# Unsplit attention scores beside the first chunk, scores of reversed sign, and other start addresses of the first layer's operands

## The chip, the cores and the metric

One NeuronCore of one Trainium2 chip. TensorE (PE in the profile, PEld its weight loads) multiplies, VectorE (DVE) and ScalarE (ACT) do everything elementwise, GpSimd (POOL) builds masks and issues transfers, SyncE (SP) issues the transfers of weights and output. The metric is the device time in microseconds (us) of one launch.

## The reference

Windowed attention with four sink keys, then two feed-forward layers on the same 1536 tokens:

```python
scores = scale * np.matmul(q, k.transpose(0, 1, 3, 2))        # batch 2, 8 heads, 768 positions, head size 64
keep = is_sink | in_window                                    # 4 sink keys, window of 128
scores = np.where(keep, scores, -1000000000.0)
scores = scores - np.max(scores, axis=-1, keepdims=True)
a = np.exp(scores)
a = a / (np.sum(a, axis=-1, keepdims=True) + 1e-09)
out = np.matmul(a, v)                                         # becomes x, 1536 x 512
h = x @ w_in                                                  # 512 x 2048
g = np.where(h >= 1, h, np.where(h <= -1, 0.0, (h + 1) ** 2 / 4))
x = g @ w_out                                                 # 2048 x 512
h = x @ w_in2
g = np.where(h > 0.0, h, np.exp(np.minimum(h, 0.0)) - 1.0)
y = g @ w_out2
```

All inputs and outputs are fp32; q and k are some 31 times larger than v, so the scores are large and the softmax is sharp.

## The kernel before

**Split operands.** A product that must be nearly exact in fp32 is made of operands rounded to TensorE's one-pass fp32 type (F32R) and their remainders: with `x_hi`, `x_lo`, `win_hi`, `win_lo` the first product of a layer is three matmuls (L510 to L512), and so is the second (L525 to L527). ACT makes a rounded part with a copy (CAST), DVE the remainder with a subtraction.

**Chunks.** The first layer runs over 6 chunks of 256 tokens, the second over 3 chunks of 512. A chunk has 16 tiles `t` of 128 hidden units. In tile `t` PE does `hidden(t)` (12 matmuls into `h_ps`), then `outward(t - 2)` (12 matmuls into `y_ps`); ACT and DVE make `ramp`, `g_full`, `g_hi` and `g_lo` from `h_ps`. In a first-layer matmul the moving operand (x or g) has 256 columns.

**Attention.** Chunk 0's attention is done first, alone (the `first_*` functions), in plain fp32. After that the attention of chunk c+1 is done beside the first layer of chunk c: the table BESIDE puts the scores of heads 0 to 7 at the ends of tiles 2, 3, 5, 6, 8, 9, 11 and 12, the exponentials one tile later, the transposes two tiles later, and the values of a pair of heads three tiles after its second head. For every head, ACT copies `k_hi` and `q_parts` (L596, L597), DVE subtracts `k_lo` and the low half of `q_parts` (L787, L788), and only then PE may run the four score matmuls (L463, L464), which wait for the semaphore qk_lo_ready. In `q_parts` the upper 64 rows hold the rounded q and the lower 64 its remainder, so a matmul with 128 rows covers both. DVE adds the mask and takes the maximum (L800), negates it (L803), and ACT uses that as the bias of the exponential (L606). DVE then normalises (L808 to L814), PE transposes the probabilities (L473, L479), ACT copies them (L611), and PE multiplies by the values (L493, L495).

**Weights.** The first layer's 16 pieces of weights are split once: three while the first attention runs (SPLITS_ALONE), the other thirteen beside chunk 0, piece 3+t at the end of tile t, each by one ACT copy (L647) and one DVE subtraction (L845) of 1024 columns. The second layer's weights are split beside chunk 5 and the first second-layer chunk.

**Order.** Every engine works through its own instruction list in order, and semaphores join them. Within a tile DVE does: the remainder split of this tile's head, the normalising of the last one, `g_lo`, `g_full`, the maximum, the sinks' split, the weights' split. POOL issues the loads of q and k of head h once the head two before it has been split (L378), which frees the buffer.

**Where things lie.** Tiles in SBUF are placed one behind the other. All that stands ahead of `small` is a multiple of 256 bytes long, `small` is 64 bytes and `half` 128. The change's title counts from a line of 256 bytes; by those sizes x begins 64 bytes into a line, and so does g, in the kernel before. The weights begin 128 bytes into one, the second layer's x and g 192.

Of the kernel before, what the change touches and what calls it, by code (L numbers as in the profile page):

```python
# [26 lines left out]
ALU = mybir.AluOpType  # L27
ACT = mybir.ActivationFunctionType

P = 128  # L30
# [21 lines left out]
LOWEST = -3.0e38  # L52
# [29 lines left out]
def build(nc, qk_first, v_first, q_t, k_t, v_w, v_s, w_in, w_out, ident_d, out, n_sink, window):  # L82
# [8 lines left out]
    with ExitStack() as ctx:  # L91
# [50 lines left out]
        behind = sb("behind", [P, 64])  # L142
# [11 lines left out]
        first_scores, first_max, first_neg_max, first_exp = sem("first_scores"), sem("first_max"), sem("first_neg_max"), sem("first_exp")  # L154
        first_sum, first_inv, first_probs, first_probs_t = sem("first_sum"), sem("first_inv"), sem("first_probs"), sem("first_probs_t")
        first_copied, first_attn = sem("first_copied"), sem("first_attn")
        qk_loaded = [sem(f"qk_loaded{n}") for n in range(4)]
        v_loaded = [sem("v_loaded0"), sem("v_loaded1")]
# [10 lines left out]
        max_done, neg_max_ready, sum_done, inv_ready, probs_ready = sem("max_done"), sem("neg_max_ready"), sem("sum_done"), sem("inv_ready"), sem("probs_ready")  # L169
# [40 lines left out]

        def begins(c, n):

            return isinstance(c, int) and c == 1 and n == 0
# [117 lines left out]
        def _(pool):  # L331
# [40 lines left out]

            def load_head(c, h):
                if isinstance(c, int) and c == 1 and h < 2:

                    pool.wait_ge(first_scores, h + 2)
                else:
                    pool.wait_ge(qk_lo_ready, heads_before(c, h) - 1)  # L378
                for to, src in zip((ks[:, h % 2, :], qs[:, h % 2, :]), (k_t, q_t)):
                    pool.dma_start(to, src[bass.ds(heads_before(c, h), 1)].rearrange("o p n -> (o p) n")).then_inc(qk_loaded[h % 4], 16)  # L380
# [16 lines left out]
            load_head(1, 0)  # L397
            load_head(1, 1)
# [4 lines left out]
            for h in range(2, HEADS):  # L403
                load_head(1, h)
                if h > 2 * 2 and h % 2 == 1:
                    load_values(1, h // 2)
# [14 lines left out]
        def _(pe):  # L421
# [43 lines left out]

            def transposes(c, h):
                p, hh = h // 2, h % 2
# [3 lines left out]
                start = hh * (SW + NS)  # L471
                for n, (j, col) in enumerate(((0, start), (0, start + P), (1, start), (1, start + P))):
                    last = pe.transpose(t_ps[:, n * P:(n + 1) * P], probs[:, j, col:col + P], ident[:, :])  # L473
                last.then_inc(probs_t_ready, 1)
                if hh == 1:
# [56 lines left out]
            def layer_chunk(layer, c, attend=None):  # L532
                for t in range(FT):
# [3 lines left out]
                    if attend is not None:  # L537
# [4 lines left out]
                        for h in BESIDE[0][t]:  # L542
                            scores(attend, h)
# [23 lines left out]
        def _(act):  # L567
            def first_exponents(p):
                banks = flight[p % IN_FLIGHT][0]
                act.wait_ge(first_neg_max, p + 1)  # L570
                if p >= IN_FLIGHT:
                    act.wait_ge(first_probs_t, 2 * (p - IN_FLIGHT + 1))
                for hh in range(2):
                    for j in range(QB):
                        nc.scalar.activation(seen_probs(p, hh)[:, SEEN_OF[j]], banks[hh][:, SEEN_OF[j]], ACT.Exp,
                                             bias=tops[:, p % IN_FLIGHT, hh, j:j + 1],
# [14 lines left out]
            def split_head(c, h):  # L591

                act.wait_ge(qk_loaded[h % 4], (heads_before(c) // 4 + (h // 4 + 1)) * 32)
                if not begins(c, h):
                    act.wait_ge(scores_ready, heads_before(c, h) * QB)
# [3 lines left out]
            def exponent(c, h):  # L599
                p, hh = h // 2, h % 2  # L600
                if hh == 0 and not begins(c, p):
                    act.wait_ge(probs_t_ready, pairs_before(c, p) * 2)
                    act.wait_ge(sinks_t_ready, pairs_before(c, p))
                act.wait_ge(neg_max_ready, heads_before(c, h) + 1)
                for j in range(QB):
                    nc.scalar.activation(probs[:, j, hh * SW:(hh + 1) * SW], s_ps[j][:, 0:SW], ACT.Exp, bias=top[:, hh, j:j + 1],  # L606
                                         accum_out=total[:, hh, j:j + 1]).then_inc(exp_done, 1)
# [377 lines left out]
```

## Time and profile before

| what | us |
|---|---|
| three runs | 638.13, 638.5, 640.57 |
| median | 638.5 |
| the profiled execution's own time | 640.01 |
| its span, first to last instruction | 638.3 |
| its granted clock | 1.000 (the upper level, 2.4 GHz) |
| PE busy / DVE busy / ACT busy | 618.0 / 339.7 / 387.9 |
| POOL busy | 74.4 |

The profiled execution is 1.5 us above the median of the runs and 1.7 us above its own span. Times in the rows count from the first instruction. Of that span the first 24.0 us are the attention of chunk 0, 24.0 to 371.1 the first layer's six chunks, and the rest the second layer. "Idle before" is the time in which an engine stood still ahead of an instruction, with the instruction that ended it. Matmuls overlap, so the length of one says little; the distance from one start to the next is its price.

### The profile page before, as it was taken

To read this page: it belongs to the slowest core of one execution; us is meant where nothing else is said; L and a number is where in the kernel's file an instruction comes from. 1 tells how busy PE (TensorE), PEld (TensorE's weight loads), DVE (VectorE), ACT (ScalarE), POOL (GpSimd) and SP (SyncE) were. 2 spreads that over 40 slices of the span, in tenths; PEclk is the share of its full clock that TensorE was granted. 3 is DMA by queue.
4 is the path that set the end of the run, shared out by engine and by line. 5 is a ranking of instruction groups with operands and counts; after the bars stand their busy time and mean duration, and the time that the engine had idled before them with its cause. 6 is when DMAs were issued, how large, how long until landed. Compare 5 with 4: busy or idle time off the path is not lost.

```text
span 638.3 us, 12201 instructions
## 1 busy us (share of the span) xinstructions
PE 618.0 (97%) x4164; PEld 552.0 (86%) x4164; DVE 339.7 (53%) x899; ACT 387.9 (61%) x926; POOL 74.4 (12%) x147
## 2 busy tenths in 40 slices
PE   5799999999999999999999999999999999999997
PEld 3688899999999999999999988888888888888886
DVE  6799958766775677487646653222332222322221
ACT  5888877776886787787767764333443334533333
POOL 5213212221221223023000000000000000000000
PEclk9999999999999999999999999999999999999999
DMA  8664212320321222123054500000100000100001
GB/s 280 223 217 142 81 41 66 106 67 27 102 89 40 64 89 89 40 64 104 0 192 145 193 1 0 2 0 1 66 0 0 0 1 1 66 0 0 0 0 66
DMA packets 15276, 42.49 MB, mean 67 GB/s; under 512 B 2852, under 2 KB 4536, under 8 KB 15248
## 3 DMA queue, kind: packets, MB, share of 16 engines
q0 software_dynamic: 7040, 20.57, 10.5%
q1 hardware_dynamic: 8208, 21.56, 9.7%
q8 instruction: 15, 0.25, 0.1%
q14 instruction: 13, 0.11, 0.1%
HBM read 38.98 MB, written 3.15 MB: 66 GB/s over the span
## 4 chain that ended last, share of the span: by engine, by line
PE 85%; DVE 7%; ACT 4%; issue 2%; DMA 0%; ACTq 0%; SPq 0%; DVEq 0%
PE h_ps L510 13%; PE h_ps L512 12%; PE h_ps L511 12%; PE y_ps L525 9%; PE y_ps L527 9%; PE y_ps L526 9%; PE s_ps L525 3%; PE s_ps L527 3%; PE s_ps L526 3%; PE o_ps L493 3%; PE t_ps L473 2%; DVE wout_lo L845 1%; PE s_ps L463 1%; PE s_ps L464 1%; DVE win_lo L845 1%
## 5 line engine op out<-in xcount | busy, mean ns | idle before, releaser
L510 PE MATMUL h_ps<-x_hi,win_hi 128*128 128x256 f32 (+1 forms) x576 | 185.7, 322 | 0.8 <-DVE g_full L869 0.3
L512 PE MATMUL h_ps<-x_hi,win_lo 128*128 128x256 f32 (+1 forms) x576 | 182.3, 317 | 0.0
L511 PE MATMUL h_ps<-x_lo,win_hi 128*128 128x256 f32 (+1 forms) x576 | 181.6, 315 | 0.0
L525 PE MATMUL y_ps<-g_hi,wout_hi 128*128 128x256 f32 (+1 forms) x480 | 145.8, 304 | 1.8 <-DVE g_lo L858 1.8
L527 PE MATMUL y_ps<-g_hi,wout_lo 128*128 128x256 f32 (+1 forms) x480 | 144.9, 302 | 0.0
L526 PE MATMUL y_ps<-g_lo,wout_hi 128*128 128x256 f32 (+1 forms) x480 | 144.3, 301 | 0.0
L510 PEld LDWEIGHTS h_ps<-x_hi,win_hi 128*128 128x128 f32 x576 | 108.3, 188 | 9.3 <-DVE g_full L869 1.2
L512 PEld LDWEIGHTS h_ps<-x_hi,win_lo 128*128 128x128 f32 x576 | 108.8, 189 | 8.4
L511 PEld LDWEIGHTS h_ps<-x_lo,win_hi 128*128 128x128 f32 x576 | 108.3, 188 | 8.0
L873 DVE SCALAR_TENSOR_TENSOR g_full<-g_full,h_ps 128x512 f32<-128x512 f32 x48 | 33.0, 687 | 151.9 <-ACT g_full L680 151.9
L858 DVE TENSOR_TENSOR g_lo<-g_full,g_hi 128x256 fp32r<-128x256 f32 (+1 forms) x144 | 73.7, 512 | 52.9 <-ACT g_hi L665 52.2
L678 ACT ACTIVATE ramp<-h_ps 128x512 f32<-128x512 f32 x48 | 28.7, 597 | 117.5 <-PE h_ps L512 116.9
L665 ACT CAST g_hi<-g_full 128x256 fp32r<-128x256 f32 (+1 forms) x144 | 68.4, 475 | 50.2 <-DVE g_full L873 34.1
L525 PEld LDWEIGHTS y_ps<-g_hi,wout_hi 128*128 128x128 f32 x480 | 90.2, 188 | 7.1 <-DVE g_lo L858 1.4
L527 PEld LDWEIGHTS y_ps<-g_hi,wout_lo 128*128 128x128 f32 x480 | 90.9, 189 | 4.2
L526 PEld LDWEIGHTS y_ps<-g_lo,wout_hi 128*128 128x128 f32 x480 | 90.2, 188 | 4.0
L869 DVE SCALAR_TENSOR_TENSOR g_full<-h_ps,ramp 128x256 f32<-128x256 f32 x96 | 40.3, 420 | 21.4 <-ACT ramp L675 21.3
L606 ACT ACTIVATE probs<-s_ps,small 128x260 f32<-128x260 f32 x80 | 37.3, 470 | 20.3 <-DVE small L803 20.3
L673 ACT ACTIVATE ramp<-h_ps,half 128x256 f32<-128x256 f32 x96 | 45.4, 473 | 5.3 <-PE h_ps L512 4.8
L380 POOL DMA_DIRECT2D ks<-in_k x40 | 22.1, 551 | 207.5 <-DVE q_parts L788 205.8
L675 ACT ACTIVATE ramp<-ramp 128x256 f32<-128x256 f32 x96 | 40.1, 418 | 3.0
L525 PE MATMUL s_ps<-g_hi,wout_hi 128*128 128x512 f32 x96 | 37.8, 394 | 0.0
(110 smaller groups left out, 814.3 us busy)
## 6 DMA issues: line engine op xcount, KB each, us to landing
ks<-in_k POOLq DMA_DIRECT2D x40, 260.0 KB, 2.9
raw<-in_w_in SPq DMA_DIRECT2D x11, 512.0 KB, 4.0
raw<-in_w_out SPq DMA_DIRECT2D x11, 512.0 KB, 4.1
qs<-in_q POOLq DMA_DIRECT2D x40, 128.0 KB, 2.8
vals<-in_v POOLq DMA_DIRECT2D x20, 192.0 KB, 3.0
out_y<-xy SPq DMA_DIRECT2D x12, 256.0 KB, 2.1
xy<-in_w_in SPq DMA_DIRECT2D x5, 512.0 KB, 5.2
xy<-in_w_out SPq DMA_DIRECT2D x5, 512.0 KB, 4.1
```

Of the source, the lines that this page charges most:

```text
L510: pe.matmul(o, win_hi[:, k, f], x_hi[:, k, :], start=(k == 0), stop=False)
L511: pe.matmul(o, win_hi[:, k, f], x_lo[:, k, :], start=False, stop=False)
L512: last = pe.matmul(o, win_lo[:, k, f], x_hi[:, k, :], start=False, stop=(k == KT - 1))
L525: pe.matmul(o, wout_hi[:, t, cols], g_hi[:, t % GR, :], start=begin, stop=False, skip_group_check=True)
L526: pe.matmul(o, wout_hi[:, t, cols], g_lo[:, t % GR, :], start=False, stop=False, skip_group_check=True)
L527: last = pe.matmul(o, wout_lo[:, t, cols], g_hi[:, t % GR, :], start=False, stop=(t == FT - 1), skip_group_check=True)
L606: nc.scalar.activation(probs[:, j, hh * SW:(hh + 1) * SW], s_ps[j][:, 0:SW], ACT.Exp, bias=top[:, hh, j:j + 1], accum_out=total[:, hh, j:j ...
L665: nc.scalar.copy(g_hi[:, t % GR, :], g_full[:, t % 2, :]).then_inc(g_hi_ready, 1)
L673: nc.scalar.activation(ramp[:, t % 2, :], h, ACT.Relu, bias=half[:, 0:1], scale=0.5).then_inc(ramp_ready, 1)
L675: nc.scalar.activation(ramp[:, t % 2, :], ramp[:, t % 2, :], ACT.Square).then_inc(bent_ready, 1)
L858: nc.vector.tensor_tensor(g_lo[:, t % GR, :], g_full[:, t % 2, :], g_hi[:, t % GR, :].bitcast(F32), ALU.subtract).then_inc(g_lo_ready, 1)
L869: nc.vector.scalar_tensor_tensor(g, h, 1.0, ramp[:, t % 2, :], ALU.max, ALU.min).then_inc(g_ready, 1)
```

## The change

Three things are changed.

1. Beside chunk 0, the attention (of chunk 1) is done in *units* in place of heads. A unit is one block of 128 queries (j) of both heads of a pair. Its scores are two plain fp32 matmuls with 64 rows each (`unit_scores`), straight from the loaded q and k; nothing is split. q and k come as pairs of heads (`in_q_pairs`, `in_k_pairs`), so four loads of q and four of k take the place of eight. The maximum, exponentials, normalising, transposes and copies are those of a head, with the roles of j and hh exchanged. Beside chunks 1 to 4 heads are split as before. ACT's and DVE's `split_head(1, 0)` ahead of chunk 0 is gone.
2. The scaled scores get the reversed sign: the reduction takes the minimum, the exponential has scale -1, and the instruction that negated the maximum (L765, L803) is gone, everywhere.
3. `half` is 32 bytes longer, and 192 bytes (`beyond_x`) lie between `x_lo` and `g_hi`: x now begins 96 bytes into a line of 256, g 32. `behind` grows by 256 bytes so that the second layer's x and raw weights still lie behind all of the first layer's tiles; their place in a line stays.

```diff
-        half = sb0("half", [P, 32])
+        half = sb0("half", [P, 40])
         x_hi, x_lo = sb0("x_hi", [P, KT, CT], F32R), sb0("x_lo", [P, KT, CT], F32R)
+        beyond_x = sb0("beyond_x", [P, 48])
...
-        behind = sb("behind", [P, 64])
+        behind = sb("behind", [P, 128])
...
+            def load_pair(p):
+                if p < 2:
+
+                    pool.wait_ge(first_scores, p + 2)
+                else:
+                    pool.wait_ge(qk_lo_ready, 2 * (p - 1))
+                for to, src in zip((ks[:, p % 2, :], qs[:, p % 2, :]), (k_pairs, q_pairs)):
+                    pool.dma_start(to, src[p]).then_inc(pair_loaded[p % 2], 16)
...
+            def unit_scores(c, u):
+                p, j = u // 2, u % 2
+                pe.wait_ge(pair_loaded[p % 2], (p // 2 + 1) * 32)
+                if not begins(c, u):
+                    pe.wait_ge(exp_done, heads_before(c, u) * QB)
+                for hh in range(2):
+                    dims = slice(HD * hh, HD * (hh + 1))
+                    pe.matmul(s_ps[hh][:, 0:SW], qs[dims, p % 2, j * P:(j + 1) * P], ks[dims, p % 2, j * SW:(j + 1) * SW],
+                              start=True, stop=True).then_inc(scores_ready, 1)
...
                 for h in BESIDE[0][t]:
-                    if h > 0:
+                    if h > 0 and not in_units(c):
                         split_head(c, h)
...
-            split_head(1, 0)
             layer_chunk(0, 0, 1, splits_first)
...
-                        nc.vector.tensor_tensor_reduce(seen, seen, mask[:, SEEN_OF[j]], SCALE, LOWEST, ALU.add, ALU.max,
+                        nc.vector.tensor_tensor_reduce(seen, seen, mask[:, SEEN_OF[j]], -SCALE, HIGHEST, ALU.add, ALU.min,
                                                        tops[:, p % IN_FLIGHT, hh, j:j + 1]).then_inc(first_max, 1)
-                dve.wait_ge(first_max, (p + 1) * 2 * QB)
-                at_once = tops[:, p % IN_FLIGHT, :, :]
-                nc.vector.tensor_scalar(at_once, at_once, -1.0, None, ALU.mult).then_inc(first_neg_max, 1)
```

PE's list in tile 5 of chunk 0, from the transposes of head 1 (unit 1) to the next tile's first matmul, before:

```order
L473 MATMUL t_ps<-ident,probs 128x128 [waits probs_t_copied,probs_ready]
L473 MATMUL t_ps<-ident,probs 128x128 x3
L479 MATMUL o_ps<-ident,probs 8x128 x2
L463 MATMUL s_ps<-k_hi,q_parts 128x260 [waits exp_done,qk_lo_ready]
L464 MATMUL s_ps<-k_lo,q_parts 128x260
L463 MATMUL s_ps<-k_hi,q_parts 128x260
L464 MATMUL s_ps<-k_lo,q_parts 128x260
L510 MATMUL h_ps<-x_hi,win_hi 128x256 [waits g_ready,w_lo_ready,w_hi_ready]
```

and the same place in the changed kernel:

```order
L502 MATMUL t_ps<-ident,probs 128x128 [waits probs_t_copied,probs_ready]
L502 MATMUL t_ps<-ident,probs 128x128 x3
L508 MATMUL o_ps<-ident,probs 8x128 x2
L492 MATMUL s_ps<-ks,qs 128x260 [waits exp_done,pair_loaded1]
L492 MATMUL s_ps<-ks,qs 128x260
L539 MATMUL h_ps<-x_hi,win_hi 128x256 [waits g_ready,w_lo_ready,w_hi_ready]
```

The four split matmuls are now two, and the wait for DVE's split has become a wait for the load.

DVE's list at the same place, from the weights' split at the end of tile 4 to the one at the end of tile 5, before:

```order
L845 TENSOR_TENSOR wout_lo<-xy,wout_hi 128x1024 [waits w_hi_ready]
L787 TENSOR_TENSOR k_lo<-ks,k_hi 128x520 [waits qk_hi_ready]
L788 TENSOR_TENSOR q_parts<-qs,q_parts 64x256
L858 TENSOR_TENSOR g_lo<-g_full,g_hi 128x256 [waits g_hi_ready]
L869 SCALAR_TENSOR_TENSOR g_full<-h_ps,ramp 128x256 [waits bent_ready]
L800 ISA s_ps,small<-s_ps,mask 128x260 [waits scores_ready]
L800 ISA small 128x1
L800 ISA s_ps,small<-s_ps,mask 128x260 [waits scores_ready]
L800 ISA small 128x1
L803 TENSOR_SCALAR small<-small 128x2 [waits max_done]
L820 TENSOR_TENSOR sinks_t<-o_ps,sinks_t 8x256 [waits sinks_hi_ready]
```

and in the changed kernel:

```order
L874 TENSOR_TENSOR wout_lo<-xy,wout_hi 128x1024 [waits w_hi_ready]
L887 TENSOR_TENSOR g_lo<-g_full,g_hi 128x256 [waits g_hi_ready]
L898 SCALAR_TENSOR_TENSOR g_full<-h_ps,ramp 128x256 [waits bent_ready]
L828 ISA s_ps,small<-s_ps,mask 128x260 [waits scores_ready]
L828 ISA small 128x1
L828 ISA s_ps,small<-s_ps,mask 128x260 [waits scores_ready]
L828 ISA small 128x1
L849 TENSOR_TENSOR sinks_t<-o_ps,sinks_t 8x256 [waits sinks_hi_ready]
```

The two subtractions between the weights' split and `g_lo`, and the negation behind the maxima, are gone.

## Rows read from the trace of the kernel before

**Rows 1.** The page's part 1: busy us, share of the span, instructions

```profile
PE 618.0 (97%) x4164; PEld 552.0 (86%) x4164; DVE 339.7 (53%) x899; ACT 387.9 (61%) x926; POOL 74.4 (12%) x147
```

**Rows 2.** Chunks 0, 1, 5: stretch, us, PE busy (x), clock, DMA share, GB/s

```profile
24.01:89.98 65.97, 61.42 (x510) 1.00 0.43 137
89.98:148.75 58.77, 58.44 (x510) 1.00 0.24 71
...
324.75:371.14 46.39, 45.70 (x387) 1.00 0.49 172
```

**Rows 3.** Waits of PEld in chunk 0 (24.01:89.98): us in total, times, longest

```profile
PEld s_ps L463 <- DVE q_parts L788: 5.4, 7, 1.3
...
PEld y_ps L525 <- DVE wout_lo L845: 0.6, 1, 0.6
```

**Rows 4.** Busy PE, PEld, DVE, ACT, POOL: three tiles of chunk 0, of chunk 1

```profile
46.55:60.05 13.50, 12.40 (x104) 11.39 (x104) 12.28 (x34) 11.95 (x31) 3.28 (x6) 1.00 0.47 157
...
109.65:121.34 11.69, 11.69 (x105) 11.20 (x104) 8.96 (x31) 9.34 (x28) 3.22 (x6) 1.00 0.31 90
```

**Rows 5.** Groups by form, 46.55 to 60.05: the split of a head, ACT then DVE

```profile
L596 ACT CAST k_hi<-ks 128x520 fp32r<-128x520 f32 x2 | 1.2, 624 | 0.0
...
L597 ACT CAST q_parts<-qs 128x256 fp32r<-128x256 f32 x2 | 0.8, 404 | 0.0
...
L787 DVE TENSOR_TENSOR k_lo<-ks,k_hi 128x520 fp32r<-128x520 f32 x2 | 1.4, 694 | 0.0
...
L788 DVE TENSOR_TENSOR q_parts<-qs,q_parts 64x256 fp32r<-64x256 f32 x2 | 0.8, 422 | 0.0
```

**Rows 6.** Timeline of PE in tile 5 of chunk 0: start us, us, instruction

```profile
41.83 0.38 PE L479 MATMUL o_ps<-ident,probs 128*8 128x128 f32 x2
43.13 0.39 PE L463 MATMUL s_ps<-k_hi,q_parts 128*128 128x260 f32 x1 [0.92 <-DVE q_parts L788]
```

**Rows 7.** Timeline of PE in chunk 4: scores after transposes, then values and scores

```profile
305.84 0.36 PE L463 MATMUL s_ps<-k_hi,q_parts 128*128 128x260 f32 x1
306.04 0.28 PE L464 MATMUL s_ps<-k_lo,q_parts 128*128 128x260 f32 x1
...
306.40 0.28 PE L510 MATMUL h_ps<-x_hi,win_hi 128*128 128x256 f32 x1
...
308.80 0.28 PE L525 MATMUL y_ps<-g_hi,wout_hi 128*128 128x256 f32 x1
...
309.23 1.09 PE L493 MATMUL o_ps<-probs_t,vals 128*64 128x256 f32 x12
310.25 0.39 PE L495 MATMUL o_ps<-sinks_t,vsink_parts 128*128 128x256 f32 x1
310.47 0.28 PE L463 MATMUL s_ps<-k_hi,q_parts 128*128 128x260 f32 x1
```

**Rows 8.** Timeline of PE, starts of matmuls: chunk 4, chunk 5, the second layer

```profile
307.10 0.28 PE L510 MATMUL h_ps<-x_hi,win_hi 128*128 128x256 f32 x1
...
310.94 0.28 PE L510 MATMUL h_ps<-x_hi,win_hi 128*128 128x256 f32 x1
...
344.93 0.28 PE L510 MATMUL h_ps<-x_hi,win_hi 128*128 128x256 f32 x1
...
351.99 0.28 PE L525 MATMUL y_ps<-g_hi,wout_hi 128*128 128x256 f32 x1
...
450.10 0.39 PE L510 MATMUL h_ps<-x_hi,win_hi 128*128 128x512 f32 x1
...
452.85 0.39 PE L525 MATMUL s_ps<-g_hi,wout_hi 128*128 128x512 f32 x1
```

**Rows 9.** Timeline at the first attention's first maximum

```profile
6.64 0.14 DVE L761 DVE_READ_ACCUMULATOR2_ANT small<- 128x1 f32 x1
...
7.12 0.37 ACT L575 ACTIVATE probs<-s_ps,small 128x128 f32<-128x128 f32 x1 [4.11 <-DVE small L765]
```

More of the change, by code:

```diff
@@ L51 @@
 MASKED = -1e9
-LOWEST = -3.0e38
+HIGHEST = 3.0e38
 SPLITS_ALONE = {0: [0], 1: [1], 2: [2]}
@@ L79, with build @@
 IN_FLIGHT = 2
-def build(nc, qk_first, v_first, q_t, k_t, v_w, v_s, w_in, w_out, ident_d, out, n_sink, window):
+def build(nc, qk_first, v_first, q_pairs, k_pairs, q_t, k_t, v_w, v_s, w_in, w_out, ident_d, out, n_sink, window):
     NS = n_sink
@@ L209, in pairs_before, with in_units, splits_before, parts_of @@
             return (c - 1) * PAIRS + p
+        def in_units(c):
+            return isinstance(c, int) and c == 1
         def begins(c, n):
-            return isinstance(c, int) and c == 1 and n == 0
+            return in_units(c) and n == 0
+        def splits_before(c, h):
+            return (c - 2) * HEADS + h
+        def parts_of(c, n):
+            return [(n % 2, hh) for hh in range(2)] if in_units(c) else [(j, n % 2) for j in range(QB)]
         size = KT * GW
@@ L402, in _ @@
             load_values(1, 1)
[L403 to L406, printed above, removed]
+            for p in range(2, PAIRS):
+                load_pair(p)
+                load_values(1, p)
             with pool.Fori(2, NC) as c:
@@ L470, in transposes @@
                     pe.wait_ge(probs_t_copied, heads_before(c, h))
-                start = hh * (SW + NS)
-                for n, (j, col) in enumerate(((0, start), (0, start + P), (1, start), (1, start + P))):
+                blocks = [(j, hh * (SW + NS) + block * P) for j, hh in parts_of(c, h) for block in range(2)]
+                for n, (j, col) in enumerate(blocks):
                     last = pe.transpose(t_ps[:, n * P:(n + 1) * P], probs[:, j, col:col + P], ident[:, :])
                 last.then_inc(probs_t_ready, 1)
-                if hh == 1:
+                if h % 2 == 1:
                     if not begins(c, p):
@@ L542, in layer_chunk @@
                         for h in BESIDE[0][t]:
-                            scores(attend, h)
+                            (unit_scores if in_units(attend) else scores)(attend, h)
                 outward(layer, c, FT - 2)
@@ L599, in exponent @@
             def exponent(c, h):
-                p, hh = h // 2, h % 2
-                if hh == 0 and not begins(c, p):
+                p = h // 2
+                if h % 2 == 0 and not begins(c, p):
                     act.wait_ge(probs_t_ready, pairs_before(c, p) * 2)
                     act.wait_ge(sinks_t_ready, pairs_before(c, p))
[L604 to L607, printed above, removed]
+                act.wait_ge(max_done, (heads_before(c, h) + 1) * QB)
+                for n, (j, hh) in enumerate(parts_of(c, h)):
+                    nc.scalar.activation(probs[:, j, hh * SW:(hh + 1) * SW], s_ps[n][:, 0:SW], ACT.Exp, scale=-1.0,
+                                         bias=top[:, h % 2, n:n + 1], accum_out=total[:, h % 2, n:n + 1]).then_inc(exp_done, 1)
             def copy_probs_t(c, h):
                 act.wait_ge(probs_t_ready, heads_before(c, h) + 1)
-                nc.scalar.copy(probs_t[:, h % 2, :], t_ps[:, :]).then_inc(probs_t_copied, 1)
+                if in_units(c):
+                    half_of_both = probs_t[:, :, h % 2 * 2 * P:(h % 2 + 1) * 2 * P]
+                    nc.scalar.copy(half_of_both, t_ps[:, :].rearrange("p (h n) -> p h n", h=2)).then_inc(probs_t_copied, 1)
+                else:
+                    nc.scalar.copy(probs_t[:, h % 2, :], t_ps[:, :]).then_inc(probs_t_copied, 1)
                 if h % 2 == 1:
@@ L811, in normalise @@
                 dve.wait_ge(inv_ready, heads_before(c, h) + 1)
-                for j in range(QB):
+                for n, (j, hh) in enumerate(parts_of(c, h)):
                     v = probs[:, j, hh * SW:(hh + 1) * SW]
-                    nc.vector.tensor_scalar(v, v, total[:, hh, j:j + 1], None, ALU.mult).then_inc(probs_ready, 1)
+                    nc.vector.tensor_scalar(v, v, total[:, h % 2, n:n + 1], None, ALU.mult).then_inc(probs_ready, 1)
             def split_sinks(c, h):
@@ L827, in before_layer @@
                 for h in BESIDE[0][t]:
-                    if h > 0:
+                    if h > 0 and not in_units(c):
                         split_head(c, h)
```

58 lines of the change are left out of this document (28 added, 30 removed).

## The prediction

> **What bounds the kernel now.** I read the page first, then the windows chunk by chunk, then the waits of PE's weight loads inside the one chunk that stands out, and last PE's timeline. The page says that PE is busy for 97% of the span, and DVE and ACT for 53% and 61% [rows 1]. So time can be won in three places only: where PE waits, in what PE is given to do, and in the distance from one matmul to the next. The windows show where it waits. Chunks 0 and 1 give PE the same 510 instructions, but chunk 0 takes 65.97 us and chunk 1 58.77 [rows 2]: 7.2 us of chunk 0 are waits. The waits view names them: 5.4 us in seven waits of the first score matmul for DVE's `q_parts` (L788), the longest 1.3, and 0.6 in one wait for DVE's `wout_lo` [rows 3]. The cause is in the windows of three tiles: beside chunk 0 DVE is busy for 12.28 of 13.50 us and ACT for 11.95, since they split weights too; beside chunk 1 the same three tiles take 11.69 us, PE is busy for all of them, and DVE has 8.96 and ACT 9.34 to do [rows 4]. DVE and ACT set the pace of chunk 0, PE that of the others. One such wait: the transposes' last part starts at 41.83, the scores behind it at 43.13 [rows 6], 1.30 later.
>
> **The change part by part.**
>
> *The splits of q and k beside chunk 0 go.* Per head that is 624 + 404 ns of ACT and 694 + 422 ns of DVE [rows 5]. Three tiles hold two heads: DVE's 12.28 us become 12.28 - 2 x 1.12 = 10.0, ACT's 11.95 - 2 x 1.03 = 9.9, against PE's 11.69 [rows 4]. Both are then below PE, and PE sets the pace of chunk 0 as in the others. What PE waited for, q_parts, isn't made any more: **-5.4 us** [rows 3]. The new wait is for the load of a pair. POOL issues pair 2 once units 0 and 1 have their maxima (tile 3) and pair 3 behind the values of pair 2, whose own wait ends in tile 6; they are needed in tiles 8 and 11, two tiles and more (over 7 us at 11.69 for three) later, so I cost it at nothing. Queued behind that wait on PE would be the whole next tile. Of the other 1.8 us of waits (7.2 - 5.4), the 0.6 for `wout_lo` comes from the same overload; the rest is the start of the chunk, where three engines go through ramp, g and the split of weights by turns, and stays. I take **-0.5**, between 0 and -1.
>
> *The scores' own price on PE.* Four split matmuls take 0.56 us from start to start where transposes stand ahead (305.84 to 306.40) and 0.47 behind values (310.47 to 310.94) [rows 7, 8]. Three of the eight heads are of the first kind. The trace has no fp32 matmul with 64 rows at the upper clock that stands alone; the nearest are the values, also plain fp32, also two side by side: twelve instructions, four of 256 columns and eight of 128, in 1.02 us (309.23 to 310.25) [rows 7]. In pairs that is 1024 columns, 1.0 ns each. A unit is four such instructions of 260 columns in pairs, 520 columns: 0.52. A change between plain fp32 and split matmuls costs time on both sides: from 308.80 to 309.23 there are three matmuls of 0.113 and 0.09 more, from 310.25 to 310.47 one and 0.11 more [rows 7]. So a unit costs between 0.52 and 0.72. Upper end: 5 x (0.72 - 0.47) + 3 x (0.63 - 0.56) = +1.5; lower end, no such edge anywhere: 5 x 0.05 - 3 x 0.04 = +0.1. I take **+0.9**, a little above the middle, because the values' rows show both edges each time.
>
> The Trainium skill, "FP8 and Floating Point Precision", section "TensorE Precision Notes", has true fp32 take four passes through the array; four of 260 columns at 2.4 GHz are 0.43 us a unit as an estimate, with which this term would be +0.2; the values' row (1.0 ns a column) speaks for more.
>
> *The pace behind the scores.* The same matmul has two paces. From 307.10 to 308.80 fifteen take 1.70 us, 113.3 ns each; from 344.93 to 351.99 sixty take 7.06, 117.7 ns each [rows 7, 8]. Nothing is waited for in either, and the clock is 1.00 in both [rows 2]. Followed through the timeline, the quick pace comes where a longer gap has stood behind plain fp32 transposes, the slow one behind split scores. Of the first layer's 2304 matmuls with 256 columns some 1200 run at the slow pace by their starts, among them all of chunk 5. In chunk 0 about 120 slow ones (five tiles of 24) follow scores alone; a unit ends like the transposes do, which would make them quick: 120 x 4.4 ns = 0.5. I take **-0.3**.
>
> *The reversed sign.* The negation of the first maximum lies on the way to the first exponential: 6.64 + 0.14 is the end of the maximum, 7.12 the start of ACT [rows 9]. Without it ACT starts some 0.3 earlier, and the first attention is a chain, so **-0.3** (0 to -0.7, if a later one counts as well). Beside the layers the negations are on DVE, which has 2.7 us to spare in three tiles [rows 4]: nothing, covered by PE's matmuls.
>
> *The new start addresses.* They touch every moving operand of the 2304 matmuls and so their pace, whose mean now is (1104 x 113.4 + 1200 x 117.7) / 2304 = 115.6 ns. If all become quick: 1200 x 4.4 ns = -5.3 us. If all become slow: 1104 x 4.4 = +4.9. The trace holds two other placings. The second layer's x and g begin 192 bytes into a line, and twelve matmuls of 512 columns take 2.75 us (450.10 to 452.85 [rows 8]), 114.6 ns for 256 columns. The scores' four moving blocks begin in four different places (k_hi 128 and 144 bytes into a line, k_lo 160 and 176), and take 0.47 for four of 260 columns, 117.5 each, 115.8 without the 1.7 ns of four columns at 2.4 GHz. The mean of these two is 115.2, or 2304 x -0.4 ns = **-0.9 us**; the ends -5.3 and +4.9 are kept.
>
> **Sum.** -5.4 - 0.5 + 0.9 - 0.3 - 0.3 - 0.9 = -6.5 us. On the profiled execution's own 640.0 that is 633.5; it stood 1.5 above the median, so against the median of 638.5 I forecast **632.0**.
>
> **The rivals.**
> - *The placing makes all matmuls quick* (-5.3 in place of -0.9): 627.6. For it: the quick pace is a stable one that the same instructions hold for whole tiles. Against: nothing says that 96 and 32 bring it about.
> - *The placing makes all slow* (+4.9): 637.8. For it: chunk 5, where nothing disturbs PE, runs slow throughout (46.39 us for 387 instructions, 120 ns each with its two gaps [rows 2]).
> - *The stalls only move.* DVE's 10.0 and ACT's 9.9 of 11.69 are busy time; each wait between them adds. If ACT and DVE again end last, at `g_lo` or `wout_lo` instead of q_parts, half of the 5.4 comes back: 634.7.
> - *Slower than before:* a start off the present grid may make a matmul dearer than either pace. The scores' second and third matmul, one of which begins 32 bytes past a multiple of 64 as x and g now will, stand 0.12 us apart (306.04 to 306.40 is three steps [rows 7]). At 120 ns for all 2304: 2304 x 4.4 = +10.1, less the other terms (-5.6): 643.0. It ends slower than before once a matmul costs over 2.4 ns more than now, 118.0.
> - *The steps drop to the floor:* with no loss between matmuls, 256 columns at 2.4 GHz are 106.7 ns; if the new places remove what makes 113 out of it, to halfway (110), 2304 x -5.6 = -12.9 instead of -0.9: 620.0. The Trainium skill, "TensorE: Matmul & The Clock Gate", section "Back-to-back issue gap", gives columns / 2.4 + 2.5 ns, 109.2 here, and by that this case would be 618.2. The trace disagrees at both paces and in the second layer.
>
> **How the numbers follow.** Forecast 0.42, all quick 0.25, all slow 0.15, stalls move 0.10, slower 0.05, floor 0.03. The likeliest gives 632.0, by itself 629.5 to 634.5. The range of 625 to 638 takes in the quick case with its own spread and the slow one, and leaves out the last two and the tails. A measurement of this kernel can tell some 0.5% (3.2 us) from no change: faster means below 635.3, slower above 641.7. Faster: nearly all of the forecast and the quick case, the floor, half of the moved stalls, 0.76; within: the slow case and the other half, 0.18; slower 0.06.
>
> **What would show each step.** Chunk 0's window should shrink from 65.97 to about 60; the waits there shouldn't name the scores, nor `ks` loads; DVE and ACT in three tiles of it should show some 10 us of 11.7. From the start of a unit to the next tile's first matmul there should be 0.5 to 0.75. The other chunks' windows change by the pace alone: 58.8 now, 56.8 if all is quick, 60 if slow, and chunk 5's 46.39 would fall to 44.8. The second layer (267 us) should stay. I am wrong if chunk 0 keeps over 63 us, or if chunk 1 moves by more than 2 us, where the addresses would outweigh everything else.

## The result and the profile after

In eleven executions of each kernel the changed one took 643.27 us in the median (641.02 to 649.91), the one before 638.5 (637.99 to 641.74): a ratio of 1.0065, 95% interval 1.0043 to 1.0087. The forecast was 632.0, in a range of 625 to 638: wrong in size and in sign. The profiled execution took 641.91 us, 1.9 more than that of before, and its span, 640.1 us, is 1.8 longer. The page's part 1, which answers to [rows 1]:

```profile
PE 624.7 (98%) x4164; PEld 556.0 (87%) x4164; DVE 324.9 (51%) x839; ACT 382.5 (60%) x910; POOL 69.1 (11%) x139
```

DVE lost 60 instructions and 15 us, as it should. ACT lost the 16 copies of the split, 8.2 us by [rows 5], but only 5.4 us of busy time: neighbours overlap in the profile, so an instruction's length isn't what its going saves. PE has as many instructions as before and is busy for 6.7 us more. Where, the windows tell (stretch, its length, PE busy with its matmuls, granted clock, DMA share, GB/s), of before the start, chunks 1 to 4 together and the second layer (chunks 0 and 5 are in [rows 2]), then of after the start, chunk 0, chunks 1 to 4, chunk 5 and the second layer.

```profile
0.00:24.01 24.01, 13.34 (x88) 1.00 0.75 261
...
89.98:324.75 234.77, 233.69 (x2035) 1.00 0.22 68
...
371.14:638.28 267.14, 263.84 (x1154) 1.00 0.03 12
```

```profile
0.00:24.37 24.37, 14.61 (x88) 0.93 0.77 263
24.37:87.73 63.36, 62.53 (x512) 1.00 0.35 115
87.73:326.27 238.54, 237.73 (x2035) 1.00 0.22 67
326.27:372.83 46.56, 45.89 (x387) 1.00 0.49 172
372.83:639.98 267.15, 263.94 (x1155) 1.00 0.03 12
```

Chunk 0 gave 2.6 us (some 5.5 to 6 were forecast), chunks 1 to 4, in which PE is given the same instructions and only start addresses and DVE's negations are changed, cost 3.8, chunk 5 (46.39 before [rows 2]) 0.2, the second layer nothing. The start has its own disturbance: its clock is 0.93.

The waits of PE's weight loads in chunk 0, all that reach 0.4 us (total, times, longest), against [rows 3]:

```profile
PEld h_ps L539 <- issue: 3.2, 10, 0.3
PEld o_ps L524 <- issue: 0.7, 4, 0.2
PEld s_ps L492 <- issue: 0.7, 3, 0.2
PEld y_ps L554 <- DVE wout_lo L874: 0.6, 1, 0.6
PEld y_ps L554 <- issue: 0.4, 1, 0.4
```

The 5.4 us for q_parts are gone, and none for a pair's load came. The 0.6 for `wout_lo` has stayed. What stands first now has no releaser and comes ten times, 0.3 us each: an edge between kinds of matmul, of which more below. Three tiles of chunk 0, with two units (busy PE, PEld, DVE, ACT, POOL), against [rows 4]:

```profile
43.30:55.88 12.58, 12.58 (x106) 11.08 (x104) 9.82 (x27) 10.53 (x27) 2.14 (x4) 1.00 0.52 174
```

DVE has 9.8 us to do (10.0 forecast), ACT 10.5 (9.9, from which the lengths of the splits had been taken in full), and PE sets the pace, busy for all 12.58. But 12.58 isn't the 11.69 of a chunk without splits: PE itself had more to do.

Where the extra time of chunks 1 to 4 is, PE's timeline shows. The first and the last of 24 layer matmuls of one tile in chunk 1:

```profile
128.66 0.28 PE L539 MATMUL h_ps<-x_hi,win_hi 128*128 128x256 f32 x1
...
131.38 0.28 PE L556 MATMUL y_ps<-g_hi,wout_lo 128*128 128x256 f32 x1
```

Those are 23 steps in 2.72 us, 118.3 ns each. Counted over all of chunks 1 to 4, the mean step from one layer matmul to the next was 115.5 ns before (quick and slow ones mixed) and is 118.1 now: 2.6 ns more on some 1480 such steps is the 3.8 us.

### The profile page after: what moved, and what is told of

It is laid out like the page before. It is cut to its first block, busy times and chain, and to the rows that moved or that the text cites. A ratio compares the mean times of both kernels' runs of the same rounds, so it can differ in the third digit from the quotient of the medians.

```text
span 640.1 us, 12174 instructions
## 1 busy us (share of the span) xinstructions
PE 624.7 (98%) x4164; PEld 556.0 (87%) x4164; DVE 324.9 (51%) x839; ACT 382.5 (60%) x910; POOL 69.1 (11%) x139
## 4 chain that ended last, share of the span: by engine, by line
PE 94%; ACT 2%; DVE 1%; issue 1%; DMA 0%; ACTq 0%; SPq 0%; DVEq 0%
PE h_ps L539 14%; PE h_ps L541 13%; PE h_ps L540 13%; PE y_ps L554 10%; PE y_ps L556 10%; PE y_ps L555 10%; PE s_ps L554 3%; PE s_ps L556 3%; PE s_ps L555 3%; PE o_ps L522 3%; PE t_ps L502 3%; PE s_ps L482 1%; PE s_ps L483 1%; PE o_ps L524 1%; PE s_ps L492 1%
## 5 line engine op out<-in xcount | busy, mean ns | idle before, releaser
L828 DVE CUSTOM_DVE_ANT_0 s_ps<-s_ps,mask 128x260 f32<-128x260 f32 x80 | 32.9, 453 | 10.9 <-PE s_ps L483 6.1
```

## The placing: the runs

**Each part alone.** Four runs on one chip: the change with the placing undone, the placing alone, the sign alone, and the change again. The kernel without the new starts:

```diff
-        half = sb0("half", [P, 40])
+        half = sb0("half", [P, 32])
-        beyond_x = sb0("beyond_x", [P, 48])
-        behind = sb("behind", [P, 128])
+        behind = sb("behind", [P, 64])
```

> The changed kernel with half, beyond_x and behind as they were, so that x and g begin 64 bytes into a line again; units and reversed sign stay. If the start addresses made the change slower (theory A), chunks 1 to 4 go back to 58.6 to 58.8 us from 59.5 to 59.7, chunk 0 stays near 63 or falls by up to 0.8, and the time is 3 to 4 us below the kernel before. If the units or the sign did it (theory B), chunks 1 to 4 stay at 59.5 to 59.7 and the time stays 1 to 5 us above before.

The kernel before with the opposite edit, `half` 40, `beyond_x` 48, `behind` 128:

> The kernel before with the three changed sizes alone: x 96 bytes into a line, g 32. Theory A: no first-layer matmul keeps the quick pace of 113.3 ns, chunks 1 to 4 take 59.5 to 59.7 us, and the time is 4 to 6 us above before. Theory B: chunks as before within 0.1 us and the time within 1 us.

The kernel before with the reversed sign only (the first attention's part of the edit; the later chunks' is the same):

```diff
-   nc.vector.tensor_tensor_reduce(seen, seen, mask[:, SEEN_OF[j]], SCALE, LOWEST, ALU.add, ALU.max,
+   nc.vector.tensor_tensor_reduce(seen, seen, mask[:, SEEN_OF[j]], -SCALE, HIGHEST, ALU.add, ALU.min,
...
-   nc.vector.tensor_scalar(at_once, at_once, -1.0, None, ALU.mult).then_inc(first_neg_max, 1)
...
-   bias=tops[:, p % IN_FLIGHT, hh, j:j + 1],
+   scale=-1.0, bias=tops[:, p % IN_FLIGHT, hh, j:j + 1],
```

> The kernel before with the reversed sign alone (minimum, scale -1, no negation). The first attention ends 0.3 us sooner by the changed kernel's first maximum; everything behind it as before: 638.2 us, between 637.8 and 638.6. If it costs something (the rival), the time is 1 us or more above before, and a window of the first 24 us or of chunk 0 shows it.

The changed kernel unedited:

> The changed kernel again, on the chip of the other three. Its eleven runs spread over 9 us with granted clocks of 0.992 to 1.000. If the spread is the clock in the first attention, this run's windows differ from the first profile's in the first 24 us alone (24.4 us at 0.93 there), and 24.0 or less is seen at clock 1.00; if it is the pace of matmuls, chunk windows differ by over 0.5 us.

Against the kernel before on the same chip (639.56 in 29 executions): units and sign at the old place 637.86, ratio 0.9953 (0.9928 to 0.9977); the placing alone 644.7, 1.0082 (1.0044 to 1.0119); the sign alone 638.47, 0.997 (0.9949 to 0.9992); the change 641.66, 1.0034 (1.0014 to 1.0054). So the parts have opposite signs, and the placing decides. The lowest time of each, at a clock of 0.999 or more, says the same: 637.93 before, 634.59, 643.69, 636.52, 640.79. By these the placing costs 5.8 on the one base and 6.2 on the other (5.1 and 3.8 by the medians). Chunks 0, 1 to 4 and 5 of the placing alone, and then of units and sign without it:

```profile
24.09:90.14 66.05, 61.87 (x510) 1.00 0.44 137
90.14:328.60 238.46, 237.63 (x2035) 1.00 0.23 67
328.60:375.15 46.55, 45.88 (x387) 1.00 0.50 171
```

```profile
25.71:89.10 63.39, 62.48 (x511) 0.98 0.36 112
89.10:323.72 234.62, 233.59 (x2035) 1.00 0.23 68
323.72:368.74 45.02, 44.11 (x387) 1.00 0.52 176
```

Chunks 1 to 4 take 238.5 with the new starts and 234.6 with the old, whatever else is in the kernel. In chunk 0 of the placing alone the loss is 0.1 us: DVE and ACT set the pace there, and a slower PE waits less (5.0 us for `q_parts` instead of 5.4). Once the splits are gone the placing costs in chunk 0 too. There the profile at the old place, run once more, has its first 2.5 us at half clock and then

```profile
27.90:88.59 60.69, 59.83 (x500) 1.00 0.34 108
```

which makes some 62.0 us for chunk 0 at full clock, an estimate, against 63.36 at the new place. Chunk 5 has two lengths at the old place, 46.3 to 46.4 (two profiles, [rows 2] one of them) and 44.9 to 45.0 (four); in the longer nearly all of its steps are slow, in the shorter nearly all are quick. With x at 96 and g at 32 only the longer comes up.

The sign alone did more than its place in the first attention. Its chunk 0, of which the first stretch ran at half clock:

```profile
24.87:90.23 65.36, 61.47 (x510) 0.98 0.43 132
...
24.87:27.60 2.73, 2.73 (x14) 0.50 0.53 175
```

At full clock that is some 64.0 us (an estimate: half of 2.73 less) for 65.97 before, and PE's loads wait 4.3 us for `q_parts` instead of 5.4. The reading, which no further run tests: with the splits still there DVE holds up chunk 0, and its negations cost time; without the splits it has time to spare, so this gain and that of the units are in part the same.

**Which start costs.** The places count, as above, from weights that begin 128 bytes into a line; what the runs show is the effect of each shift. All in the changed kernel, on one chip, one execution each (as built, x is at 96 and g at 32). x at 96 and g at 64 is `beyond_x` 56; x at 64 and g at 32 is `half` 32 and `beyond_x` 56; both at 0 is `half` 16, both at 128 is `half` 48, without `beyond_x`.

> The changed kernel, x 96 bytes into a line as changed, g back at 64. Chunks 1 to 4 took 238.5 us with x 96 and g 32, and 234.6 with both at 64. If the start of each moving operand acts on its own matmuls, this lies halfway, 236.5 (and the next run too, the two losses adding up to 3.9). If a matmul hands its phase on to the next, so that one kind of start is enough to end the quick pace for both, this and the next both stay at 238 to 238.5.

> The changed kernel, x back at 64 bytes, g at 32 as changed. Own effect: 236.5 us for chunks 1 to 4; handed on: 238 to 238.5.

> The changed kernel, x and g at the start of a line (0 and 0). If only multiples of 64 bytes matter, the two paces are as at 64: chunks 1 to 4 take 234.4 to 234.9 us, steps of 113 and 118 ns. If the place within the line of 256 matters, they differ by over 0.5 us; at the best every step is 113 ns, some 232.5.

> The changed kernel, x and g 128 bytes into a line, where the weights begin too. If multiples of 64 are all alike: 234.4 to 234.9 us for chunks 1 to 4. If moving operand and weights disturb each other when they begin at the same place of a line: over 236.

Two more places, both at 192 (the second layer's; `half` 64), on the same chip, and both at 80 (`half` 36), on another:

> The changed kernel with the first layer's x and g both 192 bytes into a line of 256, the place that the second layer's x and g have. Chunks 1 to 4 so far: 234.7 us with both at 64, 238.5 with 96 and 32, 239.7 with both at 0, 240.3 with both at 128. If a start carries its pace with it into any program place, the second layer's 114.5 ns per 256 columns should come here too: 1024 x 4 / 4 x 0.7 ns less than at 64 per four chunks, about 234. If odd multiples of 64 are good and even ones bad: also near 234 to 235. If 64 alone is good: 238 to 240.

> The changed kernel with the first layer's x and g both 80 bytes into a line of 256, a multiple of 16 but not of 32. Chunks 1 to 4: with both at 64 234.7, both at 192 238.0, x at 96 and g at 64 238.0. If only a multiple of 64 that is odd is good: 238 to 240. If what counts is how near the start is to 64: between 234.7 and 238. If a start off a grid of 32 is dear: over 240.

Chunks 1 to 4 of these six, in this order:

```profile
86.72:324.70 237.98, 237.10 (x2035) 1.00 0.23 67
```

```profile
89.29:326.26 236.97, 235.86 (x2034) 1.00 0.23 67
```

```profile
90.07:329.78 239.71, 238.88 (x2034) 1.00 0.23 67
```

```profile
90.54:330.88 240.34, 239.58 (x2034) 1.00 0.23 66
```

```profile
86.14:324.12 237.98, 237.10 (x2034) 1.00 0.23 67
```

```profile
87.00:325.99 238.99, 238.11 (x2035) 1.00 0.23 67
```

The whole executions took 640.25, 641.46, 645.71, 652.3, 638.45 and 647.02 us. They aren't compared as such: they hold half-clock stretches (clock 0.987 to 1.000), the two lengths of chunk 5 (45.07 with both at 192) and those of the second layer, of which below. Against 234.6 with both at 64, x alone costs 3.4 and g alone 2.4, both together 3.9: not a sum. 0 and 128 are worse than 96 and 32, so "a multiple of 64" is no rule; 192, also an odd multiple, loses 3.4, so that is none either. Of eight placings the old one is the best, and I have no rule for it. That it is the pace of 1536 matmuls and no wait shows in the PE column, which grows with the window. Nor is slow the end: with both at 128 the mean step is 119.5 ns, for 118.1 at 96 and 32.

**Is it x and g, or what lies behind them?** The pads move all later buffers too, 32 bytes lower in a line. The changed kernel with those put back:

```diff
         g_hi, g_lo = sb0("g_hi", [P, GR, CT], F32R), sb0("g_lo", [P, GR, CT], F32R)
+        beyond_g = sb0("beyond_g", [P, 8])
```

> The changed kernel with 32 bytes of pad behind the first layer's g. In the changed kernel the pads ahead of x and between x and g also move everything that lies behind g (ramp, g_full, q, k, probs, values) to 32 bytes lower in a line of 256; here x stays at 96 and g at 32, and all the rest is back where it stood before. Theory (the moving operands' own start sets the pace): chunks 1 to 4 keep 238.5 us and chunk 0 63.4. Rival (it is the buffers behind that cost, which ACT, DVE and POOL write and read): chunks 1 to 4 back near 234.7. A part of both: between.

Chunks 1 to 4 took 238.35 us, and 238.34 when it was run again, and the second layer 272.27 instead of 267.15. So of the 3.9 us at most 0.2 belong to the other buffers: x and g it is. The longer second layer was new (and the run of both at 128 had it as well), hence these three, the last with

```diff
         first_layer.close()
+        ahead = sb("ahead", [P, 32])
         g1_hi, g1_lo = sb("g1_hi", [P, GR, CT1], F32R), sb("g1_lo", [P, GR, CT1], F32R)
```

in the kernel of units and sign at the old place, so that the second layer's x and g begin at 64 instead of 192 (its other buffers move by the same 128 bytes):

> The same kernel as the run with x and g 128 bytes into a line, which took 652.3 us and showed two things at once: chunks 1 to 4 at 240.3, and a second layer 5.1 us longer than in every other trace (steps of 233 instead of 229 ns), though nothing of the second layer is placed or written otherwise there. Theory (the second layer's loss belongs to that one execution): chunks 1 to 4 again near 240.3, second layer back at 267.2, the whole near 646. Rival (it belongs to the placing, in a way I don't see): 652 again, second layer 272.3.

> The kernel with x at 96, g at 32 and all behind g back in its old place, once more, since its only execution showed the second layer at 272.3 us instead of 267.2 (648.3 in all). If that belongs to the program: all its executions near 646 to 650. If it belongs to single executions: most near 641 to 643, and one in some three to ten 5.1 higher; the profile then most likely shows 267.2.

> Units and reversed sign with the first layer's x and g at their old place (64 bytes into a line of 256), and a pad of 128 bytes ahead of the second layer's buffers, so that its x and g too begin at 64 instead of 192. In the first layer 192/192 took 239.0 us less 1.0 (59.56 a chunk) where 64/64 took 58.7, 0.9 us or 1.5% more. If the start acts alike with 512 columns: 2.1 ns off each of 1152 steps of 228.9 ns, so the second layer 267.2 becomes some 264.8, and the whole 635.5 against 637.9 for the same kernel without the pad. If 512 columns have their own reasons: 267.2 and no difference. If it does harm (the 233.5 ns steps): 272.3.

Both at 128 took 651.24 and 649.05, with the second layer at 272.26 again. The other gave 646.2 once, in the profiled execution, and 640.92 to 643.9 in the nine others. The second layer of that profile, and of the one with `ahead`:

```profile
371.74:644.00 272.26, 268.95 (x1154) 1.00 0.03 12
```

```profile
368.61:640.87 272.26, 268.97 (x1154) 1.00 0.03 12
```

So the second layer has two lengths, 267.2 and 272.3, to a tenth alike in every trace, with nothing waited for in either. Which comes up can change from one execution of a program to the next: none of the five profiles with the first layer at 64 and the second untouched has the longer one, six of the thirteen with another first layer have it. The program has a share in it even so: all three executions with both at 128 are that long by their times. With the second layer's own start at 64 the times lie higher, by 5.0 at the lowest and 4.4 in the median (639.23 to 642.63 against 634.22 to 639.09, on the same chip): I expected a gain of 2 and got the ratio 1.0005 (0.9981 to 1.0029) to before instead of 0.995. By its distance of 5.1 from 641.1 at full clock, the changed kernel's 646.23 is most likely such an execution; its 649.91, at clock 0.994, may be one. What picks the length is open.

## The unit's price: the runs

**What a unit costs on PE.** The timeline of PE in the changed kernel, around a unit behind values (start, us, line, instruction), against [rows 7] and [rows 8]:

```profile
59.93 0.38 PE L524 MATMUL o_ps<-sinks_t,vsink_parts 128*128 128x256 f32 x1
60.24 0.71 PE L492 MATMUL s_ps<-ks,qs 64*128 64x260 f32 x4
60.88 0.39 PE L539 MATMUL h_ps<-x_hi,win_hi 128*128 128x256 f32 x1
61.11 0.28 PE L540 MATMUL h_ps<-x_lo,win_hi 128*128 128x256 f32 x1
```

and in the kernel before the last of the same steps, which begin at 310.25 [rows 7]:

```profile
311.06 0.28 PE L511 MATMUL h_ps<-x_lo,win_hi 128*128 128x256 f32 x1
```

From L524 to the tile's second matmul is 61.11 - 59.93 = 1.18 us, before 311.06 - 310.25 = 0.81. It isn't the unit alone (0.64 for 0.47): the step ahead of it is 0.31 for 0.22, and the one behind it 0.23 for 0.12. The same sum holds behind transposes and behind y (1.07 for 0.71), and at the old place as well (1.17 and 1.07): 0.36 to 0.37 more for each of eight units, **+2.9 us**. If the split's own 0.47 is added, a unit behind values or y costs 0.84. How much of that is columns, and how much edge:

```diff
+                for again in range(2):
                     for hh in range(2):
...
-                              start=True, stop=True).then_inc(scores_ready, 1)
+                                        start=True, stop=True)
+                        if again:
+                            one.then_inc(scores_ready, 1)
```

> The changed kernel with both score matmuls of each of chunk 0's eight units given to PE twice (the second pair writes the same banks again; only it is waited for). The changed kernel's chunk 0 shows some 0.84 us per unit, against 0.47 to 0.56 of split scores. Theory A (the price of a unit lies in its own four instructions of 260 columns): chunk 0 grows by 8 x 0.84 = 6.7 us, 63.4 to 70. Theory B (half of it is the changes between plain fp32 on 64 rows and split matmuls, on each side): only the body comes twice, at the values' 1.0 ns a column 8 x 0.52 = 4.2 us, 67.6; at one column per cycle 8 x 0.43 = 3.5, 66.8. Chunks 1 to 4 unchanged at 238.5.

Four instructions more in the block, here ahead of the first matmul of the tile:

```profile
45.56 1.15 PE L493 MATMUL s_ps<-ks,qs 64*128 64x260 f32 x8
46.64 0.39 PE L542 MATMUL h_ps<-x_hi,win_hi 128*128 128x256 f32 x1
46.87 0.28 PE L543 MATMUL h_ps<-x_lo,win_hi 128*128 128x256 f32 x1
```

The block lasts 1.08 instead of 0.64, with the same steps ahead and behind, so the four themselves cost 0.44. That holds for all eight. Chunk 0 is at 67.69, 4.3 more, of which 1 us is clock (the first row below ran at half), so 3.3 for eight units: theory B, at its lower price. The second layer of this profile was the longer one.

```profile
25.65:27.60 1.95, 1.95 (x11) 0.50 0.88 264
27.60:93.34 65.74, 64.92 (x533) 1.00 0.32 101
```

Of 0.84 us, 0.44 are the unit's own and 0.40 stand at its edges. The Trainium skill's four passes ("FP8 and Floating Point Precision", section "TensorE Precision Notes"), 0.43 as an estimate if a unit's two matmuls run side by side, agree with the 0.44; against them I had taken the values' 1.0 ns a column, a row that probably has edges inside.

**What makes the edge.** Units ahead of values and transposes, at the old place, against the same kernel in the old order, which was run again beside the second layer's kernels, on another chip:

```diff
+                        if in_units(attend):
+                            for h in BESIDE[0][t]:
+                                unit_scores(attend, h)
                         for p in BESIDE[3][t]:
                             values(attend, p)
                         for h in BESIDE[2][t]:
                             transposes(attend, h)
-                        for h in BESIDE[0][t]:
-                            (unit_scores if in_units(attend) else scores)(attend, h)
+                        if not in_units(attend):
+                            for h in BESIDE[0][t]:
+                                scores(attend, h)
```

> Units and reversed sign with x and g at their old place, and each unit's scores ahead of its tile's values or transposes instead of behind them. A unit's two neighbours are then a split matmul and a plain fp32 one of 128 rows, as now, but in the other order. Theory R (the 0.4 us at a unit's edges comes of the change between 64 and 128 rows): it stays at both ends, 8 x 0.84 us, and chunk 0 at full clock is the same as without this edit (some 62.0 us). Theory F (it comes of the change between split and plain fp32): the edge towards the values or transposes goes and theirs towards the next tile stays what it is, 0.2 us for each of the six units with such a neighbour, 1.2 us less in chunk 0. The whole: 636 to 638 by R, 635 to 637 by F, so the window decides and not the median.

> Units and reversed sign with x and g at their old place, once more, beside the three others: 637.9 before in ten executions from 634.6 to 639.0, ratio 0.995. Expected again 0.995, with chunks 1 to 4 at 234.7 and second layer at 267.2 in every execution, no value 5 above the rest.

The old order gave 636.34, ratio 0.9952 (0.993 to 0.9974) to the kernel before on its chip; the new one 640.25, 0.9984 (0.9957 to 1.0012) on its own. PE's timeline with units first, a tile with transposes and one with values:

```profile
56.75 0.28 PE L555 MATMUL y_ps<-g_hi,wout_lo 128*128 128x256 f32 x1
56.96 0.71 PE L491 MATMUL s_ps<-ks,qs 64*128 64x260 f32 x4
57.60 0.66 PE L501 MATMUL t_ps<-ident,probs 128*128 128x128 f32 x4
58.09 0.38 PE L507 MATMUL o_ps<-ident,probs 128*8 128x128 f32 x2
58.23 0.36 PE L538 MATMUL h_ps<-x_hi,win_hi 128*128 128x256 f32 x1
58.43 0.28 PE L539 MATMUL h_ps<-x_lo,win_hi 128*128 128x256 f32 x1
...
61.02 0.28 PE L555 MATMUL y_ps<-g_hi,wout_lo 128*128 128x256 f32 x1
61.85 0.71 PE L491 MATMUL s_ps<-ks,qs 64*128 64x260 f32 x4 [0.55 <-ACT probs L637]
```

and the transposes' tile in the old order:

```profile
55.80 0.28 PE L555 MATMUL y_ps<-g_hi,wout_lo 128*128 128x256 f32 x1
...
57.31 0.39 PE L538 MATMUL h_ps<-x_hi,win_hi 128*128 128x256 f32 x1
57.53 0.28 PE L539 MATMUL h_ps<-x_lo,win_hi 128*128 128x256 f32 x1
```

From the last y to the tile's second matmul is 1.68 us with the unit first and 1.73 with it last. Theory F asked for 0.2 less, and with transposes it falls: plain fp32 stands beside plain fp32 and the edge stays. In the values' tile, the wait left out, it is 2.2 for 2.4 by the starts, so theory R doesn't hold whole either. Common to both is a change of the part of the array in use, 64*128, 128*64 or 128*128 in the rows. The Trainium skill, "TensorEngine Tiling (Array Packing)", section "Key Properties", says that a change of tiling mode drains the engine, and I had not weighed it. In the values' tile the new order has three such changes for four, and is 0.18 us shorter. In the transposes' tile it has two as before, if the sinks' part, 128*8, isn't counted, and is 0.05 shorter; with it counted, it has one change more and should be longer. So the rule fits the one tile, and the other only in part; no run takes it alone. Nor is it the whole, since an edge of 0.09 stands between plain fp32 and split matmuls of the same 128*128, where no unit is near (chunk 1 of the changed kernel; 124.59 to 124.80 is 0.21 for 0.12):

```profile
124.24 0.60 PE L502 MATMUL t_ps<-ident,probs 128*128 128x128 f32 x4
124.59 0.36 PE L539 MATMUL h_ps<-x_hi,win_hi 128*128 128x256 f32 x1
124.80 0.28 PE L540 MATMUL h_ps<-x_lo,win_hi 128*128 128x256 f32 x1
```

And the order brought a new wait: three units now wait for the exponentials that read the banks they write, some 0.6 us each, and chunk 0 took 65.23 us for 63.19 in the old order, both at clock 0.98.

## Why the prediction was wrong

**The step that failed is the one on the new start addresses** (-0.9). I bounded it rightly, at -5.3 and +4.9, and then chose a value near the middle from two placings of other instructions: 512 columns in the second layer, 260 in the scores. Neither speaks for 256 columns of x and g: put where the second layer's lie, they lost 3.4 us in four chunks. What happened is the rival "all slow", and a little more (118.1 ns a step for its 117.7): +3.8 in chunks 1 to 4, +0.2 in chunk 5 against this trace, and in chunk 0 the 1.0 that chunk 1 shows (59.73 for 58.77), together **+5.0** against its +4.9. I gave it 0.15. Its sum was made with the other terms as forecast, so it still came out at 637.8.

**The unit's price** was mis-sized: **+2.9** for +0.9, outside my +0.1 to +1.5. The mechanism, edges on both sides, was named. But I priced a unit from its start to the next matmul, which measured 0.64 and so lay inside "0.5 to 0.75", and left out the longer steps ahead of it and behind the first matmul of the tile.

**The waits** were right, and the gain a little larger: chunk 0 stood 7.2 us above chunk 1, and stands 3.6 above now, of which 2.9 are units. So 0.7 us of waits are left where 1.3 were expected: **-6.5** for -5.9. Chunk 0 is then -6.5 + 2.9 + 1.0 = -2.6. That this is the measured change proves nothing, since the -6.5 and the 1.0 are differences of the same windows; the 2.9 alone was read apart. By the old place's 62.0 the placing costs chunk 0 some 1.3 (an estimate) rather than 1.0. "The stalls only move" did not happen. That chunk 0 keeps over 63 us and chunk 1 moves were my two signs of being wrong; chunk 0 did and chunk 1 moved by 1.0, half of the bound that I set for one chunk, which was too wide a bound: four such chunks outweigh chunk 0's gain.

**The pace behind units** (-0.3) did not come, since the new placing leaves hardly any quick stretch in the first layer. At the old place it did: with units there the mean step in chunk 0 was 114.2 ns, for 116.1 before, some 0.7 us over its 384 matmuls. The term had its mechanism right and fell with the placing. The floor rival took its formula too widely: in the section that it names, "Back-to-back issue gap" of the Trainium skill's "TensorE: Matmul & The Clock Gate", it is the gap of an isolated matmul and not of a stream with weight loads. The quickest stretches here took 113.3 ns for its 109.2.

**The sign** (-0.3) was too small. The start took 23.47 in the repeated run of the change at clock 1.00, against 24.01: -0.5; in five traces of the changed kernel and its placings at clock 1.00 it took 23.39 to 23.57. Alone the sign is worth a ratio of 0.997, more than the start gives, by the 2.0 us in chunk 0 told above. That the later negations are "nothing" holds for the change as a whole, where PE sets the pace of chunk 0, and not for the sign by itself.

**From its own time to the median.** I took off the 1.5 us by which the profiled execution stood above its median. In it chunk 5 took 46.39, and 45.0 in four of the five profiles of the old place taken later (46.33 in the one with units first): so that 1.5 was most likely chunk 5's pace, which the new placing has in every trace. So 640.0 - 6.5 + 2.9 + 5.0 - 0.5 = 640.9, and nothing to take off; the repeated run's profiled execution took 640.79, its median 641.66. The 643.27 of the first result lies 1.6 higher. Its executions at clocks of 0.992 to 0.997 are seven of eleven, against four of ten, and one or two probably had the longer second layer.

**A version below both** is the one with units and sign at the old place: 0.9953 and 0.9952 of the kernel before on two chips, 634.22 in its lowest execution against 637.96 on the same chip. Of my sum without the placing, -5.6, it has 3.7.

## What to carry to other kernels

A start address inside a line of SBUF is a parameter like any other for a kernel that is bound by the steps between matmuls: here one pair of numbers costs 2.2% of their time (3.9 us of 1536 x 116 ns), nothing in the traces says why, and it has to be measured with the very instructions that use it, since neighbours in other shapes said nothing. When small matmuls of another shape are put between large ones, price them from the last large one to the second large one behind, since their edges fall outside their own rows. And where a change joins a repair with a new layout, run the two apart first; here each alone moved the time more than both together.

## What the runs showed of the hardware

- Four chunks, 1536 matmuls of 256 columns with the attention between them, take 234.6 to 240.3 us, by where x and g begin in a line of 256 bytes: best 64/64 (234.6), then 64/32 (237.0), 96/64 and 192/192 (238.0), 96/32 (238.5), 80/80 (239.0), 0/0 (239.7), 128/128 (240.3). Repeats agree within 0.2 us.
- The second layer, 1152 matmuls of 512 columns, takes 267.2 or 272.3 us and nothing between in 19 profiles (steps of 229 or 233 ns), with nothing waited for.
- A block of plain fp32 matmuls with 64 rows between split ones with 128 costs 0.40 us at its edges, nearly as much as its own four instructions (0.44). Behind plain fp32 matmuls with 128 rows the second step of a split stretch is 0.21 us instead of 0.12.
- In many executions PE's granted clock is 0.50 (1.2 GHz) for some us in the first 28, as in the row 25.65:27.60 above. It moves the start by up to 2.3 us (23.4 to 25.7) and chunk 0 by 1 to 1.4, and goes with the longer executions: of 25 of the kernel before on one chip, those at a mean clock of 0.999 or more took 637.96 to 640.26 us, those at 0.995 or less 639.93 to 643.02.
